# Attention's chunks in one loop over all units, the preparation of a batch in two parts, and loads of routing and weights in another order

## What is computed

```python
def _attn_ref(q, k, v, a_re, a_im):
    mag = np.sqrt(a_re * a_re + a_im * a_im)
    scale = np.minimum(mag, 0.999) / (mag + 1e-06)
    a_re_n, a_im_n = (a_re * scale, a_im * scale)
    for t in range(S):
        ar, ai = (a_re_n[:, :, t, :, None], a_im_n[:, :, t, :, None])
        new_re = ar * S_re - ai * S_im
        new_im = ar * S_im + ai * S_re
        kv = np.einsum('bhd,bhe->bhde', k[:, :, t], v[:, :, t])
        S_re, S_im = (new_re + kv, new_im)
        y[:, :, t] = np.einsum('bhd,bhde->bhe', q[:, :, t], S_re)

def _moe_ref(x, modality_id, w_gate, modality_bias, w1, w2):
    logits = x @ w_gate + modality_bias[modality_id]
    e_idx = np.argmax(logits, axis=1)
    ...
    h = np.maximum(x[mask] @ w1[e], 0.0)
    out[mask] = gate_w[mask, None] * (h @ w2[e])

def _moe2_ref(x, w1, w2, w3, w_out):
    return ((x @ w1) * (x @ w2) @ w3) @ w_out
```

## Time and profile before

| | |
|---|---|
| median of 3 runs | 1000.62 us (999.3 to 1003.11) |
| the profiled execution | 1000.67 us, span 998.9 |
| PE busy | 818.7 us, 82% |
| DVE busy | 502.0 us, 50% |
| ACT busy | 345.5 us, 35% |
| POOL busy | 127.1 us, 13% |
| mean granted PE clock | 0.936 of full speed |

### The profile page before, as it was taken

How to read it: one execution, slowest core, us unless ns; L and a number is a source line. 1 busy time by engine, 2 the same in 40 slices (tenths; PEclk the granted TensorE clock), 3 DMA queues, 4 the chain that set the end, 5 groups by cost and what they waited for, 6 DMA issues and landing times.

```text
span 998.9 us, 11923 instructions
## 1 busy us (share of the span) xinstructions
PE 818.7 (82%) x4617; PEld 675.6 (68%) x4617; DVE 502.0 (50%) x927; ACT 345.5 (35%) x676; POOL 127.1 (13%) x126
## 2 busy tenths in 40 slices
PE   0059500299798899898999999999999999999996
PEld 0035200168687788786788888878898989898985
DVE  2599999969688665274644544545111111111110
ACT  6921100243534433343534534534313131313120
POOL 0201100000000302220000000000323232323232
PEclk9999855599989799699999999999999999999998
DMA  9934300384636546615353335215000000000000
GB/s 382 381 125 158 106 5 0 69 225 126 176 106 165 145 120 145 222 57 147 110 158 108 113 96 159 87 48 186 1 32 1 32 1 32 1 32 1 32 1 32
DMA packets 47913, 102.95 MB, mean 103 GB/s; under 512 B 12130, under 2 KB 30307, under 8 KB 45539
## 3 DMA queue, kind: packets, MB, share of 16 engines
q1 hardware_dynamic: 41666, 81.91, 26.6%
q0 software_dynamic: 5632, 18.94, 5.5%
q10 hardware_dynamic: 544, 1.20, 0.5%
HBM read 64.06 MB, written 18.95 MB: 83 GB/s over the span
## 4 chain that ended last, share of the span: by engine, by line
PE 64%; DVE 20%; ACT 6%; DMA 4%; issue 3%; SPq 2%; POOL 0%; DVEq 0%
PE moe_bank L512 17%; PE moe_bank L514 17%; PE moe_bank L513 17%; DVE rows L930 3%; PE bank L1198 3%; PE bank L1166 3%; DVE rows L931 2%; DVE gates L933 2%; PE bank L1215 2%; PE bank L1124 2%; DVE gates L934 1%; DVE gates L920 1%; PE bank L1219 1%; DMA gates<-a_im 1%; PE bank L1174 1%
## 5 line engine op out<-in xcount | busy, mean ns | idle before, releaser
L1696 DVE TENSOR_TENSOR u_sb<-x_in,moe_bank 128x512 f32<-128x512 f32 x48 | 33.0, 688 | 229.9 <-PE moe_bank L514 229.9
L512 PE MATMUL moe_bank<-xT_hi,w_hi 128*128 128x512 f32 x288 | 114.2, 396 | 1.3 <-DVE xT_lo L482 1.3
L514 PE MATMUL moe_bank<-xT_hi,w_lo 128*128 128x512 f32 x288 | 113.7, 395 | 0.0
L513 PE MATMUL moe_bank<-xT_lo,w_hi 128*128 128x512 f32 x288 | 113.7, 395 | 0.0
L1559 POOL TENSOR_TENSOR hid_lo<-u_sb,hid_hi 128x512 fp32r<-128x512 f32 x48 | 62.4, 1300 | 386.1 <-ACT hid_hi L1605 386.1
L1137 PE MATMUL bank<-early_w_out,early_w3T 128*128 128x384 f32 x128 | 46.2, 518 | 63.3 <-DMA early_w_out<-w_out 59.9
L1129 PE MATMUL bank<-consts 128*128 128x512 f32 x36 | 18.9, 682 | 77.1 <-DVE gates L996 77.1
L1137 PEld LDWEIGHTS bank<-early_w_out,early_w3T 128*128 128x128 f32 x128 | 25.3, 202 | 83.6 <-issue 62.6
L1620 ACT COPY x_in<-moe_bank 128x512 f32<-128x512 f32 x48 | 28.2, 587 | 147.6 <-PE moe_bank L514 147.6
L512 PE MATMUL moe_bank<-hid_hi,w_hi 128*128 128x512 f32 x168 | 66.8, 397 | 4.5 <-DVE w_lo L472 3.0
L1129 PEld LDWEIGHTS bank<-consts 128*128 128x128 f32 x36 | 7.7, 222 | 86.6 <-issue 86.6
(11 more groups left out here) (182 smaller groups left out, 1758.0 us busy)
## 6 DMA issues: line engine op xcount, KB each, us to landing
stage<-w SPq DMA_DIRECT2D x14, 1536.0 KB, 7.6
ks<-mags SPq DMA_DIRECT2D x48, 144.0 KB, 3.0
x_sorted<-early_zero POOLq DMA_DIRECT2D x8, 772.0 KB, 20.0
qs<-gates SPq DMA_DIRECT2D x42, 146.2 KB, 3.1
x_in<-x_sorted SPq DMA_DIRECT2D x28, 193.0 KB, 3.6
gates<-a_re SPq DMA_DIRECT2D x4, 1170.0 KB, 12.3
gates<-a_im SPq DMA_DIRECT2D x4, 1170.0 KB, 14.6
spare<-k SPq DMA_DIRECT2D x4, 1152.0 KB, 6.0
```

The lines of the kernel that those rows point to most:

```text
L512: nc.tensor.matmul(out, l_hi, r_hi, start=first, stop=False)
L513: nc.tensor.matmul(out, l_hi, r_lo, start=False, stop=False)
L514: return nc.tensor.matmul(out, l_lo, r_hi, start=False, stop=last)
L1696: nc.vector.tensor_tensor(u_sb[:, f % 2], a_sb[:, f % 2], bank_b[f % 2][:, :], ALU.mult).then_inc(u_ready, 1)
```

## The change

- *One loop.* The loops over b, m and c become one over g = 0 to 48, all chunks of all units (`CHUNKS` = 48). In iteration g the engines work on the scores of chunk g and on state and y^T of chunk g - 1, whatever unit these belong to. A batch has 12 slots. The decay ends stand behind the scores of a unit's first chunk and the state product of the unit before. PE waits for q, v and k of a unit ahead of its first scores.
- *Two parts.* Every batch is prepared in stages of 1536 and 768 columns, at slots of their own: `norm` of the first part in slot 0, `finish` in 2 to 8; of the second part `join` in 2 to 4, `norm` in 5, `finish` in 7, 9 to 11 and, one batch on, 0 and 1; `join` for the batch after next in 8 to 10. On ACT log and exp stand in slots 1 and 2, and 6 and 7, squares in 5 and 11.
- *Loads.* SP's order goes by unit: second unit's k, v, q, then the next batch's q load, then the k, v and q of the next batch's first unit. The store of `least` comes ahead of the q stack of the first unit of batch 3, and no longer ahead of that of the second; its row load is later and has no wait behind it. w1 of the first expert is loaded ahead of the last q stack, w2 behind it, then x.
- *Routing* is done sooner by some slots: group 0 in batch 1 and 2, group 1 in batch 2, its place in slot 2 of batch 3. The rank matmuls use another bank.

```diff
-        RANKS_AT = {(r + 2) * NU: r for r in range(B - 2)}
-        RANKS_AT[B * NU - 1] = B - 2
+        RANKS_AFTER = {5 * NCH - 1: 0, 6 * NCH - 1: 1, 7 * NCH - 1: 2}
...
-        stages = [(0, slice(0, first_half)), (0, slice(first_half, GB * NCH)),
-                  *((b, slice(0, GB * NCH)) for b in range(1, B))]
+        first_part = -(-HU * D // P) * NCH
+        parts = (slice(0, first_part), slice(first_part, GB * NCH))
+        stages = [(b, part) for b in range(B) for part in parts]
```

SP's program, new (the old one is in the listing above):

```diff
+            for b in range(B):
+                sp.wait_ge(kinv_ready, 2 * b + 2)
+                if b + 1 < B:
+                    load_k(b + 1)
+                if b:
+                    sp.wait_ge(yT_psum, b * SLOTS)
+                sp.wait_ge(kt_ready, 2 * b + 2)
+                stack_k(b, 1)
+                if b:
+                    load_v(b, 1)
+                if b == B - 1:
+                    sp.dma_start(L.least_row[:, :], io["least"].rearrange("p o -> o p"),
+                                 allow_slow_non_contiguous=True).then_inc(least_in, DMA)
+                sp.wait_ge(ks_in[1], (b + 1) * (DMA * n_ks))
+                sp.wait_ge(qt_ready, 2 * b + 2)
+                if b == B - 1:
+                    sp.wait_ge(R.first_ready, 1)
...
+                stack_q(sp, b, 1)
...
+                if b + 1 < B:
+                    load_q(b + 1)
+                    sp.wait_ge(yT_psum, b * SLOTS + NCH)
+                    sp.wait_ge(kt_ready, 2 * b + 3)
+                    stack_k(b + 1, 0)
+                    load_v(b + 1, 0)
+                    if b == B - 2:
                         sp.wait_ge(least_ready, 1)
                         sp.dma_start(io["least"], L.least[:, :]).then_inc(least_out, DMA)
                         sp.wait_ge(least_out, DMA)
...
+                    sp.wait_ge(ks_in[0], (b + 2) * (DMA * n_ks))
+                    sp.wait_ge(qt_ready, 2 * b + 3)
+                    stack_q(sp, b + 1, 0)
+            sp.dma_start(L.stage2[:, :, :], io["w2"][bass.ds(e, 1)].rearrange("a (k p) f -> p (a k) f", p=P)).then_inc(W.w2_in, DMA)
             sp.wait_ge(R.sorted_early, L.groups[1][1] * DMA)
             load_x(sp, L, io, W, row)
```

DVE's and ACT's preparation, new:

```diff
+                now, first, second, after = 2 * b + 1, 2 * b + 2, 2 * b + 3, 2 * b + 4
+                if slot == 0:
+                    finish(now, 4)
+                elif slot == 1:
+                    finish(now, 5)
+                    finish(now, 6)
+                if b + 1 < B:
+                    if slot == 0:
+                        norm(first)
+                    if 2 <= slot <= 8:
+                        finish(first, slot - 2)
+                    if 2 <= slot <= 4:
+                        join(second, slot - 2)
+                    if slot == 5:
+                        norm(second)
+                    if slot == 7:
+                        finish(second, 0)
+                    if 9 <= slot <= 11:
+                        finish(second, slot - 8)
+                if b + 2 < B and 8 <= slot <= 10:
+                    join(after, slot - 8)
...
+                if b + 1 < B:
+                    if slot == 1:
+                        log(2 * b + 2)
+                    elif slot == 2:
+                        exp(2 * b + 2)
+                    elif slot == 5:
+                        squares_of(2 * b + 3)
+                    elif slot == 6:
+                        log(2 * b + 3)
+                    elif slot == 7:
+                        exp(2 * b + 3)
+                if b + 2 < B and slot == 11:
+                    squares_of(2 * b + 4)
```

More of the change, by code:

```diff
@@ L1088, in vector @@
             V.gate(B - 1)
-            V.read_rank(B - 1, rank)
+            V.read_rank(B - 1, late_rank)
             V.place(B - 1)
@@ new lines, in tensor @@
+                if g in (2, 3):
+                    keep_busy(4 if g == 2 else 2, bank_yT[(g + 1) % 2])
+                if g and last < NCH - 1:
+                    pe.wait_ge(krows_ready, before * (NCH - 1) + last + 1)
+                    if last:
+                        pe.wait_ge(state_ready, before * (NCH - 1) + last)
+                    for i in range(HU):
+                        at = (before % NU * NCH + last) * VC + i * D
+                        mm = nc.tensor.matmul(bank_s[0:SD, i * WIDE:(i + 1) * WIDE], krs[last % 2][:, i],
+                                              v_flat[:, at:at + WIDE], start=(last == 0 and i == 0), stop=True,
+                                              skip_group_check=True)
+                    mm.then_inc(sum_psum, 1)
```

406 lines of the change are left out of this document (177 added, 229 removed).

## The result

| | kernel before | changed kernel |
|---|---|---|
| median, number of runs | 999.22 us, 20 | 991.2 us, 20 |
| lowest to highest | 991.38 to 1014.41 | 986.84 to 1002.74 |
| the profiled execution | 1000.67 us, span 998.9 | 989.71 us, span 987.9 |

The ratio is 0.994, with a 95% interval of 0.9911 to 0.9968: faster by some 8 us where 17.9 were forecast. The runs of the changed kernel lie in two groups in the first comparison and in e1 (about 987 to 994 us and 996 to 1003); the nine of e16 lie between 985.65 and 991.65, with no upper group. All profiled ones are of the lower group, and so no trace here shows what makes the upper.

What follows compares the result with a forecast made beforehand. PE bounds attention at full speed, but waits at batch starts and late loads lower its clock. Summed unit times end attention at 420.1 instead of 437.97, 17.9 us off 1000.67: 982.8 us, forecast 977 to 989, over 8 in 10 within 970 to 996.

Steps and rivals of the forecast that it cites:

- the first two parts: In attention: the pipeline over all chunks and the two-part preparation at fixed slots, removing waits at starts of batches 1 and 2.
- w1 ahead of the last q stack: Last unit's loads: 1.5 MB of w1 goes out before q on the same queue; taken as hidden, costed at nothing.
- the low clock behind the store: First unit of batch 3: PE idles waiting for q, so its clock falls; 3.5 us added, between 2.5 and 4.5.
- The pipeline over all chunks: Attention: a unit's drain runs in the next unit's first chunk; a unit takes 23.9 us, against 24.6 at best before.
- the decay ends: Starts of batches 1 and 2: their matmul comes late behind ACT's squares; 0.6 us allowed at each.
- Preparation at fixed slots: Attention, per batch: vector engine needs 47 us, near 45 with overlaps, against PE's 47.8; batch-start waits and low clock go.
- Rival B: Attention: the vector engine paces, each batch with preparation running 3 to 4 us over; 993 us; chance 0.22.
- D: Rival: the loss only moves, the two batch-start waits returning inside the unit; 999 us, no change; chance 0.07.
- C: Rival: stacks come late at every unit, PE idling at each of six unit starts; 1018 us, slower; chance 0.06.
- The store of `least_col`: First unit of batch 3: the store takes 9.7 us to land, delaying q; PE waits 6.2 us.
- The tail: From attention's last value product to the end: keeps its instructions but for two weight splits, 562.7 us.
- The sum: Unit starts added up: attention ends at 420.1 instead of 437.97, 17.9 us less than 1000.67, giving 982.8 us.

Runs made afterwards that it cites:

- e1: The changed kernel as it is, run again on another chip: 995.46 us, ratio 0.9975 to the kernel before.
- e16: The changed kernel as it is, run again in the last series, on one chip with three other kernels: 988.97 us, ratio 0.9912 to the kernel before.
- e17: Changed kernel with SP's wait for the store of `least_col` moved ahead of the load of least_row, behind the next unit's k: 981.12 us, ratio 0.9824.
- e5: Changed kernel with GpSimd's scatters of groups 0 and 1 waiting until the q stack of units 6 and 7 has landed: 992.22 us, ratio 0.9938.
- e18: Changed kernel with the late wait for `least_col` and w1 loaded in two halves, one ahead of the last q stack, one behind: 978.13 us, ratio 0.9795.
- e8: Changed kernel with late wait for `least_col`, scatters waiting for q, and w1 loaded behind the last q stack, its splits later: 986.92 us, ratio 0.9858.
- e6: Changed kernel with the late wait for `least_col` and scatters of groups 0 and 1 waiting for q: 987.55 us, ratio 0.9873.
- e3: Changed kernel with w1 loaded behind the last q stack and its splits two slots later: 996.43 us, ratio 0.9976.
- e9: The kernel before, unchanged, profiled once more on another chip: 995.4 us in one run.
- e15: The kernel before, unchanged, profiled on the chip of the last series: 1001.29 us in one run.
- e7: Kernel before with the wait for the store of `least_col` and the load of least_row moved behind the last q stack: 996.74 us, ratio 0.9992.
- e10: Changed kernel with late wait for `least_col` and each scatter of groups 0 and 1 issued only when the previous landed: 987.82 us, ratio 0.9885.

## Why the prediction was right, and where it failed

The changed kernel took 991.2 us where 982.8 were forecast. The mechanisms of the first two parts and of the store came true; what failed is w1 ahead of the last q stack at no cost (5.3 us in e16), the size of the low clock behind the store (5.7 us, not 3.5), and the use of one execution of each kernel. On chips with the stop, the stop comes in place of w1's cost.

*The pipeline over all chunks* was right to a tenth. Forecast were 23.9 us per unit; units 1 to 4 start 23.93, 23.92 and 23.92 us apart. Batch 1 was forecast to start at 259.5 and batch 2 at 307.9; their first score matmuls stand at 258.86 and 306.70. The 0.6 us allowed at each start for the decay ends behind ACT's squares did not occur. One reading was off without harm: of the two waits of the earlier trace rows only the second stands behind the logarithm, the 1.52 us at 261.17 stand ahead of it, when ACT had been squaring a whole batch (258.79 to 260.92 us).

*Preparation at fixed slots* was right too. DVE's load was put at 47 us for a batch, near 45 with overlaps; it is 44.7 in 48 (259 to 307 us), and PE waits at most 0.50 us for anybody there. Rival B (the vector engine paces) and D (the loss only moves) fall with these rows, and C (the stacks come late everywhere) as well: between 210 and 355 us no unit start waits for q. Unit 0 does, 2.54 us up to 207.55, 0.9 us later than forecast.

*The store of `least_col`* was the right mechanism with two sizes off in opposite directions. It took 8.0 us, not 9.7, and the chain began 3.8 us into the unit, not 4.6, so PE waited 3.43 us, not 6.2. The low clock behind it was put at 3.5 us and costs more; that is a second term of the sum that was mis-sized. In e16 unit 6 takes 31.7 us (359.38 to 391.06); 23.9, 0.9 for ranks and 1.2 of waiting leave 5.7 for the clock. Together 9.7 was forecast, and 9.3 (3.6 and 5.7) stands in e16; taking the wait out (e17) gave 7.9. The Trainium skill gives the fixed cost of about 2.0 us in "DMA: Bandwidth & Descriptors", section "Anatomy of one DMA", for DMAs that GpSimd issues, which the prediction does not say; this store is issued by SyncE. By it the store would, as an estimate, have added next to no wait. SP's waits were 8.0 us and, in e5 without a scatter beside the store, 8.2. The measurement decides.

*w1 in front of the last q stack, costed at nothing*, is the step that failed. The reasoning took PE to ask for q only 28.2 us after unit 6 began, and let q need "less than 7 more" from 21. But its issuing took 10.8 us (e16) or 11.7 in place of 6.9, and the landing 7.7 in place of 2.7. In e16 PE waits 1.20 us and then runs half of the next 10 us or more at the low clock: unit 7 takes 31.5 us (391.06 to 422.55) where 27.4 were forecast. With the 1.2 of waiting this is 5.3 us that the sum had at zero. That w1 is the cause, two pairs of traces show: with half of w1 moved the wait goes from 3.25 to 2.29 us (e18 against e17), and with all of it moved from 1.66 to nothing (e8 against e6), where q is in 10.1 us after its stack began and not 13.5. The long issuing is not w1's alone: with w1 ahead and no scatter beside it the stack takes 8.0 and 7.2 us (e5, e6), with scatters and no w1 ahead 7.2 (e3). In the first trace and in e1 PE does not wait for q of unit 7, since the stop lets q land in time; there unit 7 takes 27.7 us, near the 27.4 of the forecast, and the excess is in unit 6 (38.7 us where 28.4 were forecast). The Trainium skill says in "DMA: Bandwidth & Descriptors", section "Queues, rings and completion order", that each DMA engine takes the descriptors of a ring in their order. The landing in 7.7 us behind w1 agrees with it.

*The stop* is not in the forecast, since the trace it was made from had none. On a chip that has it, it costs the changed kernel this much: from the start of unit 6 to the end of attention the first trace has 66.3 us (359.82 to 426.16), e16 63.2 (359.38 to 422.55). That is 3.2 us (1.9 by the trace of e1, with 65.1) and not the 4.2 of the wait plus its low clock, because q of unit 7 then has the time to land: unit 7 no longer waits for it. The kernel before has the stop as well, yet its median is the same on every chip (997.95 to 999.3 us in six comparisons). Its traces show how that can be. In e9 unit 6 takes 33.8 us with the stop, 26.9 in the first trace; but unit 7 then takes 25.7 us in place of 34.9, since q and x have landed before they are asked for, and neither PE's wait for q nor the low clock behind it is there. Units 6 and 7 together take 59.5 us with the stop (e9), 61.7 and 62.7 without it (first trace, e15). Here before gets back all that the stop takes, and the changed kernel, whose unit 7 loses less to its loads, does not. From one trace of before with the stop (e9) this is likely and not shown; that the changed kernel gained 3.1 us on the chip of e1 and 9.2 on that of e16 fits it, the 8.0 of the first comparison does not.

The third unit of before takes 31.5 or 31.6 us in three traces and 28.7 in e7 and e9. Both of these have the stop, but it need not be the reason. The wait of 1.51 or 1.52 us at 261 us is there in all five; in e7 and e9 the clock falls right behind it, in the others only at the wait of 3.15 us. In the first trace, and then in e9, where that second wait is 0.74 us:

```profile
262.00:272.00 10.00, 7.17 (x68) 6.18 (x64) 7.38 (x16) 7.52 (x9) 0.00 (x0) 0.94 0.65 165
...
262.00:272.00 10.00, 10.00 (x61) 9.22 (x58) 5.79 (x13) 6.21 (x7) 0.00 (x0) 0.53 0.58 141
```

I read it so that a slow PE lets ACT get ahead, and the second wait shrinks. At the start of batch 2 it is e7 and e15 in which the clock falls at once (0.52 from 320 to 330 us in e15), one trace with the stop and one without, and their unit takes 30.2 us in place of 31.7.

*The tail* was forecast at 562.7 us. From 426.16 us to the whole time of 989.71 it is 563.5. That the tail doesn't change was right.

*The sum, on one chip.* Held against e16 the steps are close: unit 6 at 359.4 (forecast 364.3), unit 7 at 391.1 (392.7), end at 422.6 (420.1), time of that profiled execution 985.65 (982.8). The pair e15 and e16 differs by 15.6 us. But medians differ by 9.2 in that series, 8.0 in the first comparison and 3.1 on the chip of e1. So another step failed, one that is no mechanism: the forecast subtracted 17.9 us from a single execution of 1000.67 us, which happened to lie at the median of three runs. Over 20 runs the median of before is 999.2, and the profiled executions of the changed kernel lie 1.5, 3.3 and 7.5 us below its own medians. In the first comparison 9.9 us are missing (8.0 in place of 17.9), and by its two traces they are these: unit 6 starts 4.5 us sooner than forecast, then takes 10.3 more (the stop, and the clock behind the store), unit 7 0.3 and the tail 0.9 more, together 6.9; the other 2.9 are what the two profiled executions differ from their medians. In the pair without the stop 2.3 are missing: 5.3 for w1, less some 3 because unit 6 starts 4.9 us sooner than forecast and its clock costs 2.2 more. Why single executions differ from their medians stays open, and so does what the upper group of runs loses.

## What to carry to other kernels

When a change shortens a stage, recompute for every load behind it when it is asked for; a large load that "was always hidden" was hidden by the slowness that the change removes, and one issued ahead of what the matrix engine needs next holds that back (here from 2.7 to 7.7 us). Where a load feeds work that comes later, cut it and let the urgent transfer pass between the parts. And take a profile of the kernel before on more than one chip before pricing a change at 1%: a stop that one trace doesn't have was in ten of the twenty taken here.

## What was unexpected of the hardware

- On three of the five chips of the series, and in the first trace of the changed kernel, the completion of TensorE's matmuls reached ACT and DVE late (4.7 and 4.5 us in the first trace) beside some groups of GpSimd's six scatters, in both kernels, with or without other transfers. Beside group 1, where it always came, the first late signal came 0.8 to 1.8 us behind the last scatter in nine traces of ten. On the two other chips, and in the first trace of before, the same scatters had no effect. How the one causes the other, these traces don't show; scatters issued one at a time had no stop in the one trace (e10) that could show it.
- A store of 512 bytes (one column, to DRAM) behind a k stack and a v load held its waiter for 8.0, 8.2 and 9.7 us in three kernels, with scatters beside it or not.
- A wait of 1.2 us for q was followed by a stretch of 10 us at a granted clock of 0.60, one of 3.6 us by 10 us at 0.50. So 1 us of idle PE can cost four more, but need not: the same wait of 1.5 us was followed by 10 us at 0.94 in one trace of the kernel before and at 0.53 in another.
